# Second layer in two phases: first product by quarters and by seven quarter products per chunk pair, activation kept whole in SBUF

## What is computed

```python
def _moe_ref(x, w_in, w_out, g_ln):        # 512 -> 1024 -> 512
    h = x @ w_in
    ...
    return (ln @ w_out).astype(np.float32)

def _moe2_ref(x, w_in, w_out):             # 512 -> 2048 -> 512
    h = x @ w_in
    r = np.maximum(h, 0.0)
    g = r * r
    return (g @ w_out).astype(np.float32)
```

## Time and profile before

| what | value |
|---|---|
| median of three runs | 484.2 us |
| profiled execution, first to last instruction | 481.6 us |
| PE busy | 471.1 us (98%), 2634 products |
| DVE busy | 278.1 us (58%) |
| ACT busy | 212.9 us (44%) |
| POOL busy | 103.8 us (22%) |
| products of the second layer | 576 (line 1675) and 576 (line 1689), 389 ns each |
| first one of line 1675 starts at | 204.70 us |
| last product starts at | 477.88 us |

### The profile page before, as it was taken

The page is one execution under the profiler, slowest core; times in us unless marked ns, Lnnn a source line. Parts: engine busy times, 40 slices in busy tenths (PEclk is TensorE's granted clock), DMA queues, the critical chain, the costliest instruction groups (busy, mean ns, idle before and its releaser), DMA issues.

```text
span 481.6 us, 7337 instructions
## 1 busy us (share of the span) xinstructions
PE 471.1 (98%) x2634; PEld 382.5 (79%) x2634; DVE 278.1 (58%) x514; ACT 212.9 (44%) x559; POOL 103.8 (22%) x155
## 2 busy tenths in 40 slices
PE   7889999999999999999999999999999999999997
PEld 5667787887788888878888888888888888888885
DVE  3899889898989888767755354322222233222232
ACT  3677777656777666242324253222222232222221
POOL 2366323231321232739930000000000000000000
PEclk9999999999999999999999999999999999999999
DMA  7931437765569424498400000200000020000002
GB/s 214 315 92 50 136 85 215 205 192 159 149 180 219 113 57 120 119 252 240 90 1 0 1 0 1 87 0 0 0 0 0 0 87 1 0 0 1 0 1 87
DMA packets 51990, 41.80 MB, mean 87 GB/s; under 512 B 28088, under 2 KB 38072, under 8 KB 51448
## 3 DMA queue, kind: packets, MB, share of 16 engines
q1 hardware_dynamic: 51192, 40.74, 29.9%
q10 hardware_dynamic: 768, 0.66, 0.5%
HBM read 30.38 MB, written 11.01 MB: 86 GB/s over the span
## 4 chain that ended last, share of the span: by engine, by line
PE 91%; DVE 3%; POOL 2%; ACT 1%; DMA 1%; issue 1%; ACTq 0%; DVEq 0%; POOLq 0%
PE score_ps L1675 27%; PE h_ps L1689 14%; PE w_ps L1516 13%; PE h_ps L1476 12%; PE w_ps L1689 7%; PE wt_ps L1689 7%; PE o_ps L1438 4%; PE score_ps L1404 2%; PE wt_ps L1404 2%; PE wt_ps L1415 1%; DMA x2T<-qT 1%; PE o_ps L1459 1%; POOL pT_own L576 1%; PE w_ps L1541 1%; DVE prob L1095 1%
## 5 line engine op out<-in xcount | busy, mean ns | idle before, releaser
L1675 PE MATMUL score_ps<-x2T_hi,w2in_hi 128*128 (+1 forms) x192 | 74.8, 389 | 0.0
L1675 PE MATMUL score_ps<-x2T_hi,w2in_lo 128*128 (+1 forms) x192 | 74.7, 389 | 0.0
L1675 PE MATMUL score_ps<-x2T_lo,w2in_hi 128*128 (+1 forms) x192 | 74.7, 389 | 0.0
L1328 DVE TENSOR_TENSOR e<-e 128x512 f32<-128x512 f32 x24 | 17.9, 744 | 82.0 <-ACT e L968 82.0
L1328 DVE TENSOR_TENSOR sq<-relu 128x512 f32<-128x512 f32 x24 | 17.2, 717 | 77.0 <-ACT relu L968 77.0
L968 ACT ACTIVATE relu<-score_ps 128x512 f32<-128x512 f32 x24 | 14.3, 597 | 90.5 <-PE score_ps L1675 90.5
L968 ACT ACTIVATE e<-score_ps 128x512 f32<-128x512 f32 x24 | 14.4, 599 | 89.7 <-PE score_ps L1675 89.7
L1675 PEld LDWEIGHTS score_ps<-x2T_lo,w2in_hi 128*128 128x128 f32 x192 | 36.0, 188 | 7.5
L1675 PEld LDWEIGHTS score_ps<-x2T_hi,w2in_hi 128*128 128x128 f32 x192 | 36.1, 188 | 7.5
L1675 PEld LDWEIGHTS score_ps<-x2T_hi,w2in_lo 128*128 128x128 f32 x192 | 36.0, 188 | 7.4
L742 ACT ACTIVATE prob<-sm,nbias 128x132 f32<-128x132 f32 (+1 forms) x96 | 37.6, 393 | 4.1 <-DVE nbias L1019 3.4
(11 more groups left out here) (192 smaller groups left out, 1095.0 us busy)
## 6 DMA issues: line engine op xcount, KB each, us to landing
u_dram<-uT SPq DMA_DIRECT2D x18, 256.0 KB, 3.2
lnT_raw<-u_dram SPq DMA_DIRECT2D x36, 128.0 KB, 2.9
w2in<-w_in SPq DMA_DIRECT2D x4, 1024.0 KB, 5.3
w2out<-w_out SPq DMA_DIRECT2D x8, 512.0 KB, 9.9
V<-v SPq DMA_DIRECT2D x12, 256.0 KB, 3.2
x2T<-x_dram SPq DMA_DIRECT2D x12, 256.0 KB, 4.8
x_dram<-x SPq DMA_DIRECT2D x44, 64.0 KB, 2.2
k_raw<-kT SPq DMA_DIRECT2D x20, 132.0 KB, 2.9
```

The lines of the kernel that those rows point to most:

```text
L1328: nc.vector.tensor_tensor(sq[f % 2], relu[f % 2], relu[f % 2], ALU.mult).then_inc(sq_ready, 1)
L1675: done = mm(h2_ps[f % 2], ws[:, c, fs], xs[:, c, bass.ts(blk, BLK)], start=(c == 0 and i == 0), stop=(c == MC - 1 and i == 2))
```

## The change

The 1536 tokens become two passes (s) of 768, each of two halves of 384 (TH). The 16 chunks of hidden features become 8 pairs (j): chunk j and chunk j+8. All of the activation, g, is kept in SBUF (8 x 2 x 1536 floats per partition), and the second product starts when the first is complete.

**First product.** Pairs 0 and 1 are computed by plain quarters: `quarter(n)`, 16 of them, each one chunk by one half of one pass, 12 products of 384 columns, in two banks in turn; ScalarE's `drain` copies each into g. Pairs 2 to 7 are computed by `multiply`: seven quarter products (a two by two scheme over the two chunks and the two halves of the tokens, the inner dimension halved too), 12 products of 384 columns each for both passes together. Their operands are sums and differences: of the activation (`sum_x` on VectorE, once, rounded and split by `round_x` and `split_x`) and of the weights (`sum_w2` on GpSimd, four instructions of 256 elements per pair, then `round_w2` on ScalarE and `split_w2` on GpSimd, parts of 512, 512, 512 and 256 elements). Their results are combined by adding in PSUM and by five VectorE sums per pair of 768 elements, each of a PSUM and an SBUF operand; ScalarE copies two (`copy_p1`, `corner`). relu and square are one VectorE instruction over 1536 elements (`gate_row`, `gate_block`).

**Second product.** `project2(t)` makes 48 products of 512 columns per tile of tokens. w2_out comes in eight pieces of 1024 elements (512 KB) through two raw buffers (`load_wy`, `round_wy`, `split_wy`), g is rounded and split per tile of 2048 elements (`round_g`, `split_g`). The first two tiles are interleaved by weight pieces.

**Entry.** project(9) is cut into 8 products ahead of hidden(11) and 16 behind it; w2_in comes pair by pair through two buffers.

The core of the diff:

```diff
+PASSES = 2
...
+NJ = C2 // 2
+CLASSIC = 2
+QUARTERS = ((0, 0), (1, 0), (1, 1), (0, 1))
+BLOCKS = tuple((j, s) for s in range(PASSES) for j in range(CLASSIC))
+A11, A12, S3, A22, S1, S2, S4 = range(7)
+B11, T2, B21, T3, T1, T4, B22, B12 = range(8)
+PRODUCTS = ((A11, B11, 0, True), (S2, T2, 1, True), (A12, B21, 0, False), (S3, T3, 1, False),
+            (S1, T1, 0, True), (A22, T4, 1, False), (S4, B22, 0, False))
+NP = len(PRODUCTS)
+P_FIRST, P_SECOND, P_CORNER, P_THIRD, P_LOWER, P_LEFT, P_RIGHT = range(NP)
+EARLY_TILES = 2
...
+              for j, place in enumerate((16512, 41088, 24704, 32896, 85312, 193856, 202048, 210240))]
+        g_hi = [at(52544 + i * 16384, f"g_hi{i}", [P, C2, P], F32R) for i in range(2)]
+        g_lo = [at(60736 + i * 16384, f"g_lo{i}", [P, C2, P], F32R) for i in range(2)]
+        y = [at(50304, "y0", [P, DM]), at(93504, "y1", [P, DM])]
 
 
         q_loaded, k_loaded, v_loaded = sem("q_loaded"), sem("k_loaded"), [sem(f"v_loaded{i}") for i in range(2)]
...
+            def load_w2(j):
+
+                if since(j, 2):
+                    sp.wait_ge(w2_split, w2_parts_before(j - 1))
+                for r in range(2):
+                    cols = slice((r * NJ + j) * P, (r * NJ + j + 1) * P)
+                    sp.dma_start(w2_raw[j % 2][:, :, r, :], w2_in[:, cols].rearrange("(c p) f -> p c f", p=P)
+                                 ).then_inc(w2_loaded[j % 2], 16)
+
+            def load_wy(j):
+
+                sp.wait_ge(*((wy_split, j - 1) if j >= 2 else (w2_split, w2_parts_before(NJ - 1 + j))))
+                sp.dma_start(wy_raw[j % 2][:, :, :],
+                             w2_out.rearrange("(r j p) m -> p r j m", r=2, p=P)[:, :, j, :]
+                             ).then_inc(wy_loaded[j % 2], 16)
...
-            sp.wait_ge(h_done, 2 * NT)
-            for c in range(C2 // 2):
...
+            sp.wait_ge(lnT_split, len(LN_PARTS) * (NT - 1))
+            load_w2(1)
+            load_w2(2)
             store_x2(NT - 2)
+            load_x2T(1, TPB + QH3, NT - 1, x2T_loaded[2])
             store_x2(NT - 1)
...
+            load_x2T(1, NT - 1, NT, x2T_end_loaded)
+            for j in range(3, NJ):
+                load_w2(j)
+            for j in range(NJ):
+                load_wy(j)
...
+            def sum_w2(j):
+
+                done = 4 * (j - CLASSIC)
+                pool.wait_ge(w2_loaded[j % 2], 32 * (j // 2 + 1))
+                if j == CLASSIC:
...
+                                        ).then_inc(w2_summed, 1)
+
+            def split_w2(j):
+                for i, part in enumerate(w2_order(j)):
+                    pool.wait_ge(w2_rounded, w2_parts_before(j) + i + 1)
+                    nc.gpsimd.tensor_tensor(w2_slots(w2_lo[j % 2], part), w2_part(j, part),
+                                            w2_slots(w2_hi[j % 2], part).bitcast(F32), ALU.subtract).then_inc(w2_split, 1)
...
+            def drain(n):
+
+                j, s = BLOCKS[n // len(QUARTERS)]
+                r, h = QUARTERS[n % len(QUARTERS)]
+                act.wait_ge(multiplied, n + 1)
+                nc.scalar.copy(g[:, j, r, s * TS + h * TH:s * TS + (h + 1) * TH], quarter_ps[n % 2]).then_inc(corner_ready, 1)
+
+            def copy_p1(j):
+                act.wait_ge(multiplied, multiplied_before(j) + P_FIRST + 1)
+                nc.scalar.copy(corner_of(j, 1, 0), pair_of(j, 0)).then_inc(p1_copied, 1)
...
+            def round_wy(j):
+                act.wait_ge(wy_loaded[j % 2], 16 * (j // 2 + 1))
+                act.wait_ge(multiplied, multiplied_before(NJ - 1) + (P_CORNER + 1, P_THIRD + 1, NP)[min(j, 2)])
+                nc.scalar.activation(wy[j][:, :, 0, :], wy_raw[j % 2][:, :, :], ACT.Copy).then_inc(wy_rounded, 1)
+
+            def round_g(t, part):
+                chunks = g_parts(t)[part]
+                act.wait_ge(g_ready, gates_before(NJ - 1 if len(g_parts(t)) > 1 and part == 0 else NJ))
+                if t < 2:
+                    act.wait_ge(multiplied, multiplied_before(NJ - 1) + (P_CORNER + 1, P_LEFT + 1)[t])
+                else:
+                    act.wait_ge(y_done, t - 1)
+                nc.scalar.activation(g_hi[t % 2][:, chunks, :], g_tile(t, chunks), ACT.Copy).then_inc(g_rounded, 1)
...
             round_xT(NT - 1)
             act.wait_ge(pv_done, GROUPS * NT)
-            round_x2T(0)
+            round_x(0, B11)
+            round_x(0, B21)
+            round_w2(0)
...
+            def sum_2(j):
+                dve.wait_ge(multiplied, multiplied_before(j) + P_SECOND + 1)
+                dve.wait_ge(p1_copied, j - CLASSIC + 1)
+                nc.vector.tensor_tensor(corner_of(j, 0, 1), pair_of(j, 1), corner_of(j, 1, 0), ALU.add).then_inc(added, 1)
...
+            def gate_block(n):
+                j, s = BLOCKS[n]
+                h = g[:, j, :, s * TS:(s + 1) * TS]
+                dve.wait_ge(corner_ready, len(QUARTERS) * (n + 1))
+                nc.vector.scalar_tensor_tensor(h, h, 0.0, h, ALU.max, ALU.mult).then_inc(g_ready, 1)
...
+            def split_wy(j):
+                dve.wait_ge(wy_rounded, j + 1)
+                nc.vector.tensor_tensor(wy[j][:, :, 1, :], wy_raw[j % 2][:, :, :], wy[j][:, :, 0, :].bitcast(F32),
+                                        ALU.subtract).then_inc(wy_split, 1)
...
+            split_x(0, B11)
+            split_x(0, B21)
             square_x2(NT - 3)
             hidden_max(NT - 1, 0)
             hidden_max(NT - 1, 1)
...
+            split_x(1, T4)
+            for j in range(CLASSIC, NJ):
+                sum_2(j)
+                sum_3(j)
+                if j == CLASSIC:
+                    gate_block(3)
+                lower_right(j)
+                if j == NJ - 1:
+                    split_g(0, 0)
+                    split_wy(0)
+                lower_left(j)
+                gate_row(j, 1)
+                if j == NJ - 1:
+                    split_wy(1)
+                upper_right(j)
+                if j == NJ - 1:
+                    split_g(1, 0)
+                    split_wy(2)
+                gate_row(j, 0)
+            split_wy(3)
+            split_g(0, 1)
+            split_g(1, 1)
+            for j in range(4, NJ):
+                split_wy(j)
+            for t in range(NT):
+                if t + 2 < NT:
+                    split_g(t + 2, 0)
...
-                project(n - 2, 0, 24)
+                project(n - 2, 0, 8)
                 pe.wait_ge(u_ready, 2 * n)
                 hidden(n, 0, 24)
+                project(n - 2, 8, 24)
...
+            def quarter(n):
+
+                j, s = BLOCKS[n // len(QUARTERS)]
...
+                pe.wait_ge(w2_split, 2 * j + r + 1)
+                pe.wait_ge(xc_split[s][xs[0]], 1)
...
+                if n >= 2:
+                    pe.wait_ge(corner_ready, n - 1)
...
+                    for k in range(3):
+                        ws, x = ((w2_hi, x_hi), (w2_hi, x_lo), (w2_lo, x_hi))[k]
+                        done = mm(quarter_ps[n % 2], ws[j % 2][:, 2 * r + half, cc, :], x(s, xs[half])[:, cc, :],
+                                  start=(c == 0 and k == 0), stop=(c == MC - 1 and k == 2))
+                done.then_inc(multiplied, 1)
...
+            def multiply(j, n):
+
+                wk, xk, bank, opens = PRODUCTS[n]
+                done = j - CLASSIC
+                pe.wait_ge(w2_split, w2_parts_before(j) + (1, 2, 1, 3, 2, 3, 4)[n])
+                if n == P_FIRST:
...
+                elif n == P_CORNER:
+                    pe.wait_ge(p1_copied, done + 1)
+                elif n == P_THIRD:
+                    pe.wait_ge(added, 5 * done + 1)
+                elif n == P_LOWER:
+                    pe.wait_ge(corner_ready, corners_before(j + 1))
+                elif n == P_LEFT:
+                    pe.wait_ge(added, 5 * done + 2)
+                elif n == P_RIGHT:
+                    pe.wait_ge(added, 5 * done + 3)
+                for s in range(PASSES):
...
+                    for c in range(2):
+                        for k in range(3):
+                            ws, xs = ((w2_hi, xc_hi), (w2_hi, xc_lo), (w2_lo, xc_hi))[k]
+                            last = mm(prod_pairs[j % 2][bank][:, s, 0:TH], ws[j % 2][:, wk, c, :], xs[s][xk][:, c, :],
+                                      start=(opens and c == 0 and k == 0), stop=(c == 1 and k == 2), skip_group_check=True)
+                last.then_inc(multiplied, 1)
...
+            def project2(t, first, last):
+
+                for n in range(first, last):
+                    if t < EARLY_TILES and n % 2 == 0:
+                        pe.wait_ge(wy_split, n // 2 + 1)
+                    if n == 0:
+                        pe.wait_ge(g_split, t + 1 if t < EARLY_TILES else 2 * EARLY_TILES + t - EARLY_TILES + 1)
...
+                    if t < EARLY_TILES and n == C2 - 2:
+                        pe.wait_ge(g_split, EARLY_TILES + t + 1)
+                    for k in range(3):
+                        gs, w = ((g_hi, 0), (g_hi, 1), (g_lo, 0))[k]
```

(77 more changed lines are left out.)

466 lines of the change are left out of this document (252 added, 214 removed).

## The result

| | before | changed |
|---|---|---|
| median of four runs | 483.97 us | 487.6 us (486.46 to 489.69) |
| ratio, 95% interval | | 1.0082 (1.0056 to 1.0108) |
| profiled execution: span | 481.6 us | 487.9 us |
| TensorE busy, products | 471.1 us, 2634 | 467.2 us, 2754 |

The account below looks back on a forecast made before the run. TensorE, busy 98% of the span, was taken as the bound. 481.6 - 9.6 - 0.25 + 0.45 + 1.85 + 0.75 + 0.4 + 8.5 = 483.7 us, plus 2.6: 486.3 us, 0.4% slower; range 480.0 to 490.5, the forecast's own 484.0 to 489.0.

Parts of the forecast that it names:

- 696 products of 384 columns: First product of the second layer: 696 narrower products replace 576 of 512 columns, 120.9 us against 130.5, 9.6 us saved.
- wait for xT_lo(11): Entry to the second layer: TensorE reaches hidden(11) earlier and waits for its input, 0.45 us (0 to 1.6).
- wait for lnT_lo(10): Entry to the second layer: project(10) waits for its input, delayed behind project(9) and new rounding, 1.85 us (0 to 3).
- drain(15) ahead of P_FIRST: End of the quarters: the first pair's product waits for ScalarE to empty its bank, 0.75 us.
- pair 2: First chunk pair multiplied by the seven-product scheme: gate_block(3) ahead of lower_right on VectorE makes TensorE wait 0.4 us.
- handoff, over 96 products at 0.2266: From last pair into the second product's first two tiles: TensorE waits for split weight pieces, 8.5 us (7.1 to 11.3).
- tiles 2 to 11, 479 x 0.2266 = 108.54: Rest of the second product: 10.9 us of TensorE per tile, rounding and splitting hidden, so no added time.
- small waits of before, tail: Entry's small waits in the old kernel, some 0.25 us, drop out; the tail stays as before.
- VectorE falls behind: Rival, 8%: in the chunk pairs VectorE's gates wait for GpSimd instructions and overrun five times, giving 494.8 us.
- TensorE's clock falls to 1.2 GHz in the handoff: Rival, 15%: idling before the second product lowers the clock, costing up to 6.8 us more, half taken: 489.7 us.
- half of the waits vanish: Rival, 14%: products cost columns alone, loads take 3.2 us, tile 10's chain is no later: 480.4 us, faster.
- the whole handoff hides: Rival, 6%: all weight pieces are split by the time TensorE asks at the second product's start: 477.8 us.

## Why the prediction was right, and where it was off

The forecast was 486.3 us, 0.4% slower; it is 487.6 in the first four runs and 487.35 in seven more. Its range (480.0 to 490.5) and the forecast's own (484.0 to 489.0) hold both. It called the sign with little conviction (0.52), and the mechanism is the one it named: the handoff and the entry take back what the narrower products save. Term by term, from project(9) on (196.50 to the span's end at 487.9, before 193.69 to 481.6):

| term | forecast | measured |
|---|---|---|
| 696 products of 384 columns | -9.6 | 192 x 0.1735 + 504 x 0.1743 = 121.2: -9.3 |
| wait for xT_lo(11) | +0.45 | +0.48 |
| wait for lnT_lo(10) | +1.85 | 1.96 less a product's 0.17: +1.79 |
| drain(15) ahead of P_FIRST | +0.75 | 0.96 less 0.17: +0.79 |
| pair 2 | +0.4 | +0.49 |
| handoff, over 96 products at 0.2266 | +8.5 | 30.25 - 21.75: +8.5 |
| tiles 2 to 11, 479 x 0.2266 = 108.54 | 0 | 484.53 - 374.75: +1.24 |
| small waits of before, tail | -0.25 | the rest: -0.5 |
| sum | +2.1 | 291.4 - 287.9: +3.5 |

The products: a line through 512 and 260 columns gave 0.1737 us, the quarters run at 0.1735 and the pairs at 0.1743. By the formula of the Trainium skill (TensorE: Matmul & The Clock Gate, "Back-to-back issue gap") it would be 162.5 ns; the trace does not agree, and a line through this case's own rows was the better guide. The prediction should have said that the page gives its formula for an isolated product, and for a stream of weight loads and products 131 ns at 512 columns, which the 226.6 of this case agree with even less.

The entry: both waits came as computed from the order of instructions and the durations of before. At the first pair the record names a w_lo of GpSimd, which ended at 255.71, 0.3 us before the product started, and by the code this product waits only for the pair's first w_lo, which ended at 250.16. The copy of the last quarter ended at 255.90, and the product started at 256.00 (ACT):

```profile
255.42 0.48 ACT L1107 COPY g<-score_ps 128x384 f32<-128x384 f32 x1 [1.61 <-PE score_ps L1963]
```

So drain(15) it was, as forecast; a releaser's name is that of one of several semaphores.

The pairs: no gap in pairs 3 to 7, 14.64 us each against 14.59. The rival that VectorE falls behind gave its waits beside GpSimd a price; the twelve gates of the pairs took 1.75 to 2.14 us each, so they waited 0.4 at most. In the quarters, and in gate_block(3) of pair 2, which took 2.62 us and is what made that pair's wait of 0.49, the price is real (DVE, then POOL):

```profile
248.93 2.85 DVE L1541 SCALAR_TENSOR_TENSOR g<-g 128x1536 f32<-128x1536 f32 x1
...
248.17 1.99 POOL L795 TENSOR_TENSOR w_lo<-w_raw,w_hi 128x512 fp32r<-128x512 f32 x1 [6.56 <-ACT w_hi L1100]
...
250.12 2.83 POOL L795 TENSOR_TENSOR w_lo<-w_sum,w_hi 128x512 fp32r<-128x512 f32 x1
```

against 1.75 for a gate of this size and 1.30 for such a split at their shortest. The times fit turns: the gate, begun at 248.93, has 1.62 us left when the first split ends at 250.16, and the second split, begun at 250.12, has 1.17 left when the gate ends at 251.78. The Trainium skill (SBUF — State Buffer, "SBUF: two separate sides") has one port pair that one of the two engines holds for a whole instruction; these rows agree with it.

The handoff: counted from pair 7's start (344.50 less 14.64), pieces 0 to 3 were split at 14.6, 18.4, 22.3 and 25.1 us (forecast 14.6, 18.4, 22.4, 25.3), piece 5 at 32.1 (31.65) and piece 7 at 37.9 (38.0). A load took 3.5 us in the median where I took 3.9, but the first of them in the chain took 4.57; piece 4's was still under way then, which is the likely reason. The two errors cancelled. The last digit of the handoff's 8.5 is luck for another reason: the same handoff takes 29.3 to 30.3 us from profile to profile.

**Which steps were off.** One: "From tile 2 on, a tile is 10.9 us of PE". The price of a 512-column product was taken from other operands and is 0.2292 here, 11.00 a tile, 1.2 us in all. Two: the clock. The rival "TensorE's clock falls to 1.2 GHz in the handoff" was a case apart, with 15% and 3.4 us. It happened in three of seven profiles with this handoff, and cost nothing visible there, as the next load's wait takes it up. It should have been a part of the forecast, as a frequent thing with a small price. Three: what lies around the span. I added 2.6 us to the span, as before's median of 484.2 stood to the profiled 481.6. Before's runs with both numbers show 2.1 (484.34 and 482.2), those of the changed kernel 1.8 (489.69 and 487.9). This 0.8 too much, 1.2 too little for the tiles, 0.3 for the pairs and some 0.5 at the start, which varies from run to run, leave about the 1.1 to 1.3 us that the forecast was short.

The rivals "half of the waits vanish" and "the whole handoff hides" didn't happen. What they needed the experiments show: not luck in the loads, but another order on two engines and loads that wait for nothing. That gave 9 us.

## What to carry to other kernels

When a change saves work on the engine that is the bound, walk each seam between stages piece by piece, from the order of instructions on the engines that feed it and the durations of before: here that gave each seam within 0.1 us of the profiled execution, and the seams ate the saving. A seam has more than one owner. VectorE's order and the loads' two buffers each set part of it, and mending one of them gives less than its waits add up to if a third engine's order stands behind (ScalarE's, with the clock's fall behind its wait: 1.3 to 1.5 us lost). Mend all of it; here the low clock went with the waits.
